# Attention and two MLPs on one core: first MLP layer interleaved with attention, probabilities turned by VectorE and DMA, scores copied out of PSUM, weights streamed per tile

## The reference

```python
def _attn_ref(q, k, v, tau):                  # 4 batches, 8 heads, 576 x 64, float32
    scores = (1 / sqrt(64)) * q @ k.T
    thresh = max(scores) - tau                # per row
    scores = where(scores >= thresh, scores, -1e9)
    attn = exp(scores - max(scores))
    attn = attn / (sum(attn) + 1e-09)
    return attn @ v
def _moe_ref(x, w_in, w_out, s, b):           # 2304 tokens, 512 -> 2048 -> 512
    r = maximum(x @ w_in, 0)
    return (s * (r * r) + b) @ w_out
def _moe2_ref(x, w_in, w_out):
    h = x @ w_in
    return (h / (1 + exp(-1.702 * h))) @ w_out
# result: _moe2_ref(_moe_ref(_attn_ref(...)))
```

## Time and profile before

| | |
|---|---|
| median of 3 runs | 1176.06 us |
| lowest, highest | 1174.57, 1176.89 us |
| profiled execution: span from first to last instruction | 1173.3 us |
| what lies around the span, against the median | 2.8 us |
| instructions | 18874 |
| TensorE matmul, busy | 1116.0 us (95%) |
| VectorE, busy | 642.9 us (55%) |
| ScalarE, busy | 519.1 us (44%) |
| GpSimd, busy | 305.5 us (26%) |
| moved by DMA | 45.45 MB |

### The profile page before, as it was taken

One profiled execution on the slowest core, in us unless ns is written; L12 is line 12 of the kernel. 1 busy time (PEld: TensorE's weight loads), 2 busy tenths in 40 slices (PEclk: granted clock), 3 DMA queues, 4 the chain that ended last, 5 costly groups with the idle time before them and its releaser, 6 DMA issues.

```text
span 1173.3 us, 18874 instructions
## 1 busy us (share of the span) xinstructions
PE 1116.0 (95%) x6688; PEld 1001.0 (85%) x6688; DVE 642.9 (55%) x1136; ACT 519.1 (44%) x1135; POOL 305.5 (26%) x324
## 2 busy tenths in 40 slices
PE   4799999999998999999999999899999999999998
PEld 3566666665668899999999999799999999999998
DVE  7998898989847763434434357742323233232322
ACT  3888888887863332322223233342323223232322
POOL 3867676777634400000000004420000000000000
PEclk9999999999999999999999999999999999999999
DMA  2323222222132310000000003310000000000000
GB/s 81 92 62 80 70 80 70 80 70 75 37 101 90 108 37 1 0 0 0 0 0 0 0 0 107 108 37 1 27 0 27 0 0 27 0 27 0 27 0 27
DMA packets 37931, 45.45 MB, mean 39 GB/s; under 512 B 22544, under 2 KB 25616, under 8 KB 37904
## 3 DMA queue, kind: packets, MB, share of 16 engines
q1 hardware_dynamic: 37904, 45.11, 12.6%
HBM read 40.37 MB, written 4.72 MB: 38 GB/s over the span
## 4 chain that ended last, share of the span: by engine, by line
PE 76%; DVE 11%; issue 6%; ACT 6%; SPq 0%; DMA 0%; ACTq 0%; POOL 0%; DVEq 0%
PE h_ps L271 31%; PE y_ps L372 30%; PE scores L290 6%; PE context L316 5%; DVE g_full L495 4%; PE turned L343 4%; DVE prob L430 3%; DVE neg_max L422 2%; ACT w_hi L540 2%; ACT limit L601 1%; DVE g_full L498 1%; ACT prob L596 1%; ACT gate L643 1%; DVE k_hi L464 1%; SPq L210 0%
## 5 line engine op out<-in xcount | busy, mean ns | idle before, releaser
L372 PE MATMUL y_ps<-g_hi,w_hi 128*128 128x384 f32 x768 | 258.0, 336 | 8.0 <-DVE g_lo L506 8.0
L271 PE MATMUL h_ps<-x_hi,w_hi 128*128 128x384 f32 x768 | 258.4, 336 | 6.6 <-POOL w_lo L744 5.5
L372 PE MATMUL y_ps<-g_hi,w_lo 128*128 128x384 f32 x768 | 257.3, 335 | 0.0
L372 PE MATMUL y_ps<-g_lo,w_hi 128*128 128x384 f32 x768 | 257.3, 335 | 0.0
L271 PE MATMUL h_ps<-x_hi,w_lo 128*128 128x384 f32 x768 | 256.7, 334 | 0.0
L271 PE MATMUL h_ps<-x_lo,w_hi 128*128 128x384 f32 x768 | 256.6, 334 | 0.0
L652 ACT CAST g_hi<-g_full 128x384 fp32r<-128x384 f32 x192 | 98.6, 514 | 332.7 <-PE y_ps L372 231.2
L506 DVE TENSOR_TENSOR g_lo<-g_full,g_hi 128x384 fp32r<-128x384 f32 x192 | 107.4, 559 | 224.7 <-ACT g_hi L652 224.7
L744 POOL TENSOR_TENSOR w_lo<-raw_slab,w_hi 128x1024 fp32r<-128x1024 f32 x29 | 69.2, 2388 | 367.4 <-ACT w_hi L540 367.4
L495 DVE TENSOR_TENSOR g_full<-gate 128x384 f32<-128x384 f32 x96 | 102.4, 1067 | 109.8 <-ACT gate L643 109.8
L271 PEld LDWEIGHTS h_ps<-x_hi,w_hi 128*128 128x128 f32 x768 | 144.1, 188 | 12.1 <-POOL w_lo L744 9.7
(11 more groups left out here) (46 smaller groups left out, 1111.8 us busy)
## 6 DMA issues: line engine op xcount, KB each, us to landing
q_raw<-q_t SPq DMA_DIRECT2D x64, 144.0 KB, 2.7
k_raw<-k_t SPq DMA_DIRECT2D x64, 144.0 KB, 2.8
raw_slab<-slabs_a SPq DMA_DIRECT2D x16, 512.0 KB, 3.2
raw_slab<-slabs_b SPq DMA_DIRECT2D x16, 512.0 KB, 3.2
out_t<-act SPq DMA_DIRECT2D x6, 768.0 KB, 3.5
v_sb<-v SPq DMA_DIRECT2D x32, 96.0 KB, 2.2
v_sb<-v SPq DMA_DIRECT2D x32, 48.0 KB, 2.2
consts<-tau SPq DMA_DIRECT2D x1, 0.5 KB, 2.3
```

The source lines that it names most:

```text
L271: mm = nc.tensor.matmul(bank[:, 0:TOK], wp[f][:, w], xp[:, c, :], start=(c == 0 and n == 0), stop=(c == DC - 1 and n == 2))
L372: mm = nc.tensor.matmul(y_ps[c][:, 0:TOK], wp[f][:, w], gp[:, f % 2, :], start=(f == 0 and n == 0), stop=(f == SLABS - 1 and n == 2))
```

## The change

The program is written anew around a list of 167 *slots*, one for each attention tile and 7 more. In each slot every engine does its share of the attention tile and then 0.8 half-steps of the first MLP layer, from slot 47 on (`halves_of`); a half-step is one `hidden` or one `output`. When the slots are used up (`pure_from`), the rest of the 160 steps follows. What is different in each part:

- Scores: one buffer instead of two. `row_max` is now a copy of the scores to SBUF (`s_sb`, ring of 2), scaled, with the row minimum as its accumulator. Exponent and mask read `s_sb`.
- Turning: VectorE transposes the tile in 32x32 blocks (`turn`), and SyncE moves the blocks of a head to their places with 16 DMAs (`move_blocks`). The 5 TensorE transposes and ScalarE's copies go. q comes from the host in an order of queries that makes the blocks fit.
- q and k: ScalarE rounds both (`split_q`, `split_k`); the scaling goes into `row_max`. Rings are of 2 heads, not 4.
- Reciprocal and addition of epsilon are per tile, not per head.
- Context: one instruction group per half, in slots 14 and 16 of each pair of heads; the result is split at once in `act_hi` and `act_lo`.
- MLP: 5 tiles of 460 to 462 tokens instead of 6 of 384; one `h_ps` bank while attention lasts, four after it. The square reads `h_ps` in PSUM as one operand. Slabs are not kept: each of the 160 steps loads, casts and splits its own, in rings of 2 and 4. The y banks are copied by ScalarE alone, and split at once.

```diff
+TOK = [462, 462, 460, 460, 460]
+W_RING = 4
+OUT_LAG = 2
+CONTEXT_SLOT = [14, 16]
+MLP_FROM = 47
+SLOTS = 2 * TPH * (PAIRS - 1) + CONTEXT_SLOT[1] + 1
+W_EARLY = [20, 24, 28, 32]
+def halves_by(slot):
+    return max(0, (4 * (slot - MLP_FROM + 1)) // 5)
+def halves_of(slot):
+    return range(halves_by(slot - 1), halves_by(slot))
...
 # SyncE
+            def move_blocks(h):
+                side = h % 2
+                sp.wait_ge(turned, TPH * (h + 1))
+                if h < 2:
+                    sp.wait_ge(pads_zeroed, 4)
+                else:
+                    sp.wait_ge(context_ready, 2 * (h // 2))
+                for a in range(4):
+                    n = (TPH if a < 3 else 3) * BLK
+                    for r in range(4):
+                        c = len(range(r, BLOCKS, 4))
+                        sp.dma_start(prob_t[side][BLK * r:BLK * r + BLK, 0:c, RUN * a:RUN * a + n],
+                                     blocks[side][BLK * a:BLK * a + BLK, r::4, 0:n // BLK, :]
+                                     .rearrange("p c t j -> p c (t j)")).then_inc(moved[side], 16)
+            def load_slab(n):
+                if n >= 2:
+                    sp.wait_ge(w_lo_ready, n - 1)
+                src = (slabs_a, slabs_b)[tile_of(n)[0]]
+                sp.dma_start(raw_slab[:, n % 2, :], src[n % SLABS]).then_inc(raw_loaded[n % 2], 16)
+            def mlp(u):
+                n = u // 2 + 2
+                if u % 2 == 0 and 4 <= n < STEPS:
+                    load_slab(n)
+            for slot in range(SLOTS):
+                h, t = divmod(slot, TPH)
+                if t == 0 and 2 <= h + 1 < HEADS and h >= 1:
+                    load_head(h + 1)
+                if t == 3 and 0 <= h - 1 < HEADS:
+                    move_blocks(h - 1)
...
+                for u in halves_of(slot):
+                    mlp(u)
...
 # TensorE
+            for slot in range(SLOTS):
+                if slot < TILES:
+                    scores_of(slot)
+                for u in halves_of(slot):
+                    mlp(u)
+                due = context_due(slot)
+                if due is not None:
+                    context_of(*due)
...
 # VectorE
+                nc.vector.tensor_scalar(halves(s_sb[0:m, j % 2, :]), scores[0:m, :, 0:HALF],
+                                        scale_c[0:m, :], None, ALU.mult, ALU.min,
+                                        accum_out=neg_max[0:m, j % STATS:j % STATS + 1]
+                                        ).then_inc(max_ready, 1)
...
+            def turn(j):
...
+                dve.wait_ge(normed, j + 1)
+                if t == 0 and h >= 2:
+                    dve.wait_ge(moved[h % 2], 256 * (h // 2))
+                nc.vector.transpose(blocks[h % 2][0:m, :, t, :],
+                                    prob[0:m, j % 4, :].rearrange("p (b i) -> p b i", i=BLK)
+                                    ).then_inc(turned, 1)
...
+            for slot in range(SLOTS):
+                if slot < TILES:
+                    row_max(slot)
+                if 0 <= slot - 2 < TILES:
+                    invert(slot - 2)
+                if 0 <= slot - 1 < TILES:
+                    mask(slot - 1)
+                if 0 <= slot - 3 < TILES:
+                    turn(slot - 3)
+                for u in halves_of(slot):
+                    mlp(u)
+                due = context_due(slot)
+                if due is not None:
+                    context_lo(*due)
...
 # ScalarE
+            def slab_hi(n):
+                act_eng.wait_ge(raw_loaded[n % 2], 16 * (n // 2 + 1))
+                if n >= W_RING:
+                    act_eng.wait_ge(y_step_done, n - W_RING + 1)
+                nc.scalar.copy(w_hi[n % W_RING][:], raw_slab[:, n % 2, :]).then_inc(w_hi_ready, 1)
...
+            def mlp(u):
+                n = u // 2
+                if u % 2 == 0 and n < STEPS:
+                    gate_of(n)
+                if u % 2 == 1:
+                    if n < STEPS:
+                        gated_hi(n)
+                    if n >= OUT_LAG and (n - OUT_LAG) % SLABS == SLABS - 1:
+                        store_tile(n - OUT_LAG)
+                    if W_RING <= n + 2 < STEPS:
+                        slab_hi(n + 2)
...
+            for slot in range(SLOTS):
+                h, t = divmod(slot, TPH)
+                if slot < TILES:
+                    exponent(slot)
+                if t == 0 and h + 1 < HEADS:
+                    split_q(h + 1)
+                if t == 1 and h + 1 < HEADS:
+                    split_k(h + 1)
...
+                for u in halves_of(slot):
+                    mlp(u)
+                due = context_due(slot)
+                if due is not None:
+                    context_hi(*due)
```

More of the change, by code:

```diff
@@ L59, with context_due, tile_of @@
 SLABS = D_FF // P
-TOK = 384
-TOK_TILES = TOKENS // TOK
+TOK = [462, 462, 460, 460, 460]
+OFF = [sum(TOK[:n]) for n in range(len(TOK) + 1)]
+TOK_MAX = max(TOK)
+LAYER_TILES = len(TOK)
+LAYERS = 2
+STEPS = LAYERS * LAYER_TILES * SLABS
 SLAB = 2 * D_MODEL
-LAYERS = 2
-H_RING = 4
+W_RING = 4
+OUT_LAG = 2
 ALPHA = 1.702
[L68 to L74, removed]
+CONTEXT_SLOT = [14, 16]
+MLP_FROM = 47
+SLOTS = 2 * TPH * (PAIRS - 1) + CONTEXT_SLOT[1] + 1
+HALVES = 2 * (STEPS + OUT_LAG)
+W_EARLY = [20, 24, 28, 32]
[3 more added lines that the diff above has]
+    return range(halves_by(slot - 1), halves_by(slot))
+def context_due(slot):
+    for half in range(2):
+        if slot >= CONTEXT_SLOT[half] and (slot - CONTEXT_SLOT[half]) % (2 * TPH) == 0:
+            pair = (slot - CONTEXT_SLOT[half]) // (2 * TPH)
+            if pair < PAIRS:
+                return pair, half
+    return None
+def tile_of(s):
+    layer, tile = divmod(s // SLABS, LAYER_TILES)
+    return layer, tile, s % SLABS
 def build(nc, q_t, k_t, v, tau, slabs_a, slabs_b, s, b, out_t):
@@ new lines, in context_of @@
+            def context_of(pair, half):
+                i = 2 * pair + half
+                if half == 0:
+                    pe.wait_ge(moved[0], 256 * (pair + 1))
+                    pe.wait_ge(moved[1], 256 * (pair + 1))
+                    pe.wait_ge(v_loaded, 64 * (pair + 1))
+                if i > 0:
+                    pe.wait_ge(context_lo_ready, i)
+                for c in range(KEY_CHUNKS):
+                    for side in range(2):
+                        mm = nc.tensor.matmul(context[64 * side:64 * side + 64, 0:HALF],
+                                              v_sb[:, side, c, :],
+                                              prob_t[side][:, c, half * HALF:(half + 1) * HALF],
+                                              start=(c == 0), stop=(c == KEY_CHUNKS - 1))
+                mm.then_inc(context_ready, 1)
@@ L683, in _ @@
+            for u in range(pure_from, HALVES):
+                mlp(u)
         @block.gpsimd
         def _(pool):
[L685 to L692 removed]
@@ new lines, in _ @@
+            for slot in range(SLOTS):
+                h, t = divmod(slot, TPH)
+                if 0 <= slot - 2 < TILES:
+                    norm(slot - 2)
+                if 0 <= slot - 1 < TILES:
+                    add_eps(slot - 1)
+                if t == 0 and h + 1 < HEADS:
+                    split_q(h + 1)
+                if t == 1 and h + 1 < HEADS:
+                    split_k(h + 1)
+                if slot in W_EARLY:
+                    slab_lo(W_EARLY.index(slot))
+                for u in halves_of(slot):
+                    mlp(u)
```

820 lines of the change are left out of this document (335 added, 485 removed).

## The result

The changed kernel takes **1496.28 us** (median of 4 runs, 1493.64 to 1498.36) against 1175.87 us of the kernel before on the same chip (4 runs): ratio 1.2721 [1.2701, 1.2742]. It is slower, as forecast, but 103 us over the forecast number and 36 us above the range. The profiled execution's span is 1491.8 us.

A forecast was written before the change was run, and what follows sets the result against it. The prediction took the kernel before as bound by attention on VectorE and TensorE, then MLP matmuls. For the changed kernel, attention with covered work 811 + remaining steps 556 + tile ends 14 + tail 9 + 2.8 gave 1393 us; range 1200 to 1460.

The forecast's parts named there:

- The loop through SyncE's queue: Shared stage: slab and q wait behind 16 moves on in-order SyncE; 25.3 us a head, 27.2 after a pair's odd head.
- Rival 1: VectorE binds instead of the loop through SyncE: shared head 17.4 us, total 1137 us; chance 10%.
- Rival 2: Only GpSimd's hold on VectorE instructions with two SBUF operands costs time: +98 us, total 1235 us; chance 12%.
- Rival 3: TensorE at 1.2 GHz in the shared stage, 462-column matmuls at 385 ns; total 1450 us; chance 15%.
- Matmuls: MLP on TensorE: 205 ns a matmul, 4.92 us a step, 787 us in all against 799.
- VectorE's slot: VectorE's work per attention tile, with minimum, reciprocal, mask and block transpose (0.75 us): 2.66 us a slot.
- The moves: SyncE's 16 DMAs a head, priced by v-load issues at 0.54 us each: 8.6 us, 7.8 to 9.6.
- The landings: DMA time from issue to landing: 3.2 us for a slab, 2.7 us for q.
- The context: Context on TensorE after the last move: 1.33 us, taken from 20 matmuls in 2.65 us.
- The scale: VectorE's MLP scale takes its ordinary 0.48 us at 384 columns, 0.56 at 462, without a hold by GpSimd.
- The mask: VectorE's mask: 0.82 us in its slot; in the shared loop held by GpSimd until 23.0 us, ending at 23.7.
- Cover of the weight chain: MLP after attention: slab preparation of 4.3 us hides within 4.92 by 0.6 us; tile ends cost 14 us.

The follow-up runs named there:

- e1: Changed kernel with SyncE issuing the slab of slot 5h+3 before the 16 moves instead of behind them; 1448.55 us.
- e2: e1 plus all slabs issued two slots early and the next head's q and k loads before the moves; 1389.28 us.
- e4: Changed kernel with each of the 16 moves cut in two, 32 issues with the same bytes; 1817.17 us.
- e3: e2 plus a pair's contexts in slots 16 and 18 instead of 14 and 16, first MLP slot 49 instead of 47; 1269.66 us.
- e7: Changed kernel with 24 matmuls on zeros before each pair's first context half, filling TensorE's idle time; 1498.50 us.
- e8: e3 with the MLP in 6 tiles of 384 tokens instead of 5 of 460 to 462; 1317.18 us.

## Why the prediction was right and wrong

**The sign and the mechanism hold.** "The loop through SyncE's queue", moves ahead of slab and q, is what the chain shows piece by piece, and e1, e2 and e4 move the time by it in both directions. Rival 1 (VectorE binds, 1137 us) falls: even with the order mended the kernel is at 1270. Rival 2 (only GpSimd's hold, 1235 us) falls as the account of the changed kernel; that e3 came to within 35 us of its number is luck, since e3 still has a loop over the moves beside the hold. Rival 3's sign, matmuls of 462 columns at 385 ns, is there in 109 matmuls; the contexts of the shared stage cost no time by it (e7), and for the rest its price is open.

**The step that failed is the price of a move's issue: 0.54 us in the forecast, 0.65 measured. The landings, the context half, the held scale and the matmul's constant were mis-sized too.** The sum missed by 102 us of span: start +1, heads before the MLP +42, shared heads +46, the rest +13. The terms, in the order of the prediction:

- *Matmuls.* "462/2.4 + 13 = 205 ns": the 13 ns did not stay 13. Measured are 207 ns in `hidden` and 210 in `output`. 160 steps of 5.00 us are 800 us, as much as the 799 before; the forecast had 787. That is 9 of the +13 at the end, 113 steps at 5.00 for 4.92.
- *VectorE's slot.* Forecast 2.66 us, measured 2.20 without the MLP (from one row minimum at 99.22 us to the next at 101.42): its instructions start 0.05 to 0.08 us before their forerunner's end. The block transpose was right at 0.767 (0.75). This was too dear, and hid part of the other errors.
- *The moves.* "0.54 us each", by the v issues; they took 0.65, 10.4 us a head and not 8.6: 58 us on 32 heads, 14 before the MLP and 43 beside it, and beyond the forecast's upper end of 0.60. A move is not a v load: it goes from SBUF to SBUF, over 32 partitions and in three dimensions, and the nearest row wasn't near. e4 gives the same price by the total, 0.63 us an issue. Among the terms listed here this is the largest.
- *The landings.* 4.19 and 3.9 us for slab and q, against 3.2 and 2.7 taken from a kernel without moves. The bytes alone don't explain it: the shared stage moves 107 GB/s and the last stage 106, and in the last slabs land in 3.4 to 3.5 us. Whether it is the moves just ahead of them, no run shows.
- *The context.* A misreading of the earlier trace rows: 20 matmuls in 2.65 us are one half, not two. A half is 2.65 us at full clock and 4.76 after a wait, and the forecast had 1.33. Of the +42 before the MLP, moves (1.8 us on 8 heads) are 14 and q's landing (1.2) 10; the rest is shared by the contexts and by the early slabs of slots 28 and 32, which also stand behind moves and which the forecast's loop there didn't have. No run parts these two.
- *The scale.* "The scale behind it takes its ordinary 0.48 us" was one case made into a rule. In the shared stage L438 was held for up to 2.24 us. It has a single SBUF tensor as input. The kernel before had such a case in its rows already, the cast of k, also with one input (ns least/median/most):

```profile
L464 DVE CAST k_hi<-k_raw x32: 450/814/1708, 5.5 to 307.5; 128x576 fp32r<-128x576 f32 x32
```

The Trainium skill, page SBUF — State Buffer, section "SBUF: two separate sides", has the exclusion hold for VectorE instructions in a two-port mode too, and not only for those with two SBUF inputs; the trace agrees that this one is held, with its 2.24 us. Its free time fits too: from 384 to 462 elements it grows from 0.48 to 0.52 us, 0.5 ns an element, where the product grows from 0.56 to 0.64, 1.0 ns an element, so the scale streams at twice the product's rate. For the same reason the forecast's 0.56 for its free time was too dear.
- *The mask.* Mean 1.02 us over 160, against one of 2.7 a head in the forecast's loop (21.0 to 23.7) and four at the 0.82 of its slot, 1.20: somewhat too dear.
- In the block shown above, moves (+1.8), slab (+1.0) and scale (+1.7) make 4.5 us on the forecast's 25.3, and VectorE's shorter slot takes some of it back: 28.4.
- *Cover of the weight chain,* 0.6 us: held. In the last stage TensorE waits for a slab's rest 11 times, 10.4 us in all and never over 1.0, for which the forecast had 14 us at tile ends; with 384 columns (e8) every other hidden half-step is late.

**The range** took 0.49 to 0.60 for the issues, too narrow for an instruction that was in no row, and had no term at all for longer landings, for a held scale or for a context half of twice the price.

## What to carry to other kernels

An in-order queue that only issues DMAs can be empty most of the time and still set the pace: ask for each entry what stands behind it that someone needs soon, put loads with a deadline ahead of bulk moves (107 us here), and give the consumer of the last move more time (120 us). Then ask what the buffer that the moves fill waits for: with one buffer the moves and their consumer take turns, and that loop was left over. Price a new kind of DMA by its issue, and give it a wide upper end if no row has its shape. Where two engines hold each other, a wait removed can come back as a longer hold, so look at the mean of the held instructions together with the waits.

## What the runs showed of the hardware beyond expectation

- The spacing of float32r matmuls with new weights each was 173 ns at 384 columns and 207 or 210 (mean 208) at 462, 0.451 ns a column at both, where 2.4 GHz would give 0.417. Wider tiles saved nothing on the matmuls here.
- Issuing one SBUF-to-SBUF move of 48 to 100 KB cost SyncE 0.65 us, and a slab of 512 KB from HBM behind it 0.63 (579.37 to 580.00): the bytes don't set the price of an issue. Nor is the price fixed: the issue of a slab takes between 0.33 and 0.59 us in the changed kernel.
- The hold goes both ways: GpSimd's normalization takes 0.74 us where no mask runs (at 587.03) and 1.23 beside a mask (at 590.45), a mean of 1177 ns.
- A scale with one SBUF input streamed at twice the rate of a product (0.5 against 1.0 ns an element), and GpSimd held it for up to 2.24 us.
- TensorE's granted clock was 0.50 in mid-kernel, from 99 to 111 us, when TensorE had 1.28 us of work. It was 0.55 through the context that followed (111 to 116 us), and 1.00 from there to 125 us.
